# A three-stage kernel in float32: loads and preparatory work of its first stage rearranged, and its dense stage cut into blocks of 384 tokens

## The reference

```python
# 1: gated linear attention; 4 batches, 8 heads, 768 tokens, head size 48
for t in range(S):
    state = alpha[:, :, t, :, None] * state + np.einsum('bhd,bhe->bhde', k[:, :, t], v[:, :, t])
    y[:, :, t] = np.einsum('bhd,bhde->bhe', q[:, :, t], state)
# 2: each of 3072 tokens goes to the best of 8 experts
logits = (x / (norm(x) + 1e-6)) @ (emb / (norm(emb) + 1e-6)).T / tau
out[mask] = gate_w[mask, None] * (np.maximum(x[mask] @ w1[e], 0.0) @ w2[e])   # 384 -> 1024 -> 384
# 3: dense mixture; every token goes through all 4 experts
p = domain_probs / (domain_probs.sum(-1, keepdims=True) + 1e-9)
for e in range(4):
    out += p[:, e:e + 1] * (np.maximum(x @ w1[e], 0.0) @ w2[e])               # 384 -> 1024 -> 384
```

## Time and profile before

| what | value |
|---|---|
| time, median of 3 runs | 1276.92 us (1276.18 to 1277.35) |
| the profiled execution: its time, its span | 1278.89 us, 1277.2 us |
| TensorE busy | 1210.4 us, 95% of the span |
| VectorE, ScalarE, GpSimd busy | 504.4, 397.4, 153.2 us |
| moved by DMA | 102.86 MB |
| granted TensorE clock, mean over the span | 0.976 |

### The profile page before, as it was taken

One profiled execution on the slowest core, in us unless ns is written; L12 is line 12 of the kernel. 1 busy time (PEld: TensorE's weight loads), 2 busy tenths in 40 slices (PEclk: granted clock), 3 DMA queues, 4 the chain that ended last, 5 costly groups with the idle time before them and its releaser, 6 DMA issues.

```text
span 1277.2 us, 20420 instructions
## 1 busy us (share of the span) xinstructions
PE 1210.4 (95%) x7357; PEld 1089.5 (85%) x7358; DVE 504.4 (39%) x833; ACT 397.4 (31%) x765; POOL 153.2 (12%) x184
## 2 busy tenths in 40 slices
PE   4999559999999879999999999999999999999998
PEld 4898439989989859999999999988888899999997
DVE  5999763443444242232233233234334224223321
ACT  5667414554544331121122122123222112112111
POOL 3455522232232100000000000000000000000000
PEclk9999769999999879999999999999999999999999
DMA  8777222344244233011011011011001101300000
GB/s 302 258 249 256 74 78 87 135 142 142 86 164 169 75 130 99 26 50 50 1 50 49 0 49 49 0 50 51 1 1 50 50 1 50 123 0 0 25 25 25
DMA packets 50964, 102.86 MB, mean 81 GB/s; under 512 B 7184, under 2 KB 32784, under 8 KB 50784
## 3 DMA queue, kind: packets, MB, share of 16 engines
q1 hardware_dynamic: 42304, 84.28, 19.2%
q0 software_dynamic: 3520, 10.82, 2.7%
q10 hardware_dynamic: 5088, 7.08, 1.6%
HBM read 87.42 MB, written 14.75 MB: 80 GB/s over the span
## 4 chain that ended last, share of the span: by engine, by line
PE 91%; DVE 3%; DMA 2%; issue 1%; ACT 1%; SPq 1%; POOL 0%; ACTq 0%; DVEq 0%; POOLq 0%
PE bank L763 11%; PE bank L765 11%; PE bank L764 11%; PE bank L778 10%; PE bank L780 10%; PE bank L779 10%; PE bank L672 3%; PE bank L684 3%; PE bank L686 3%; PE bank L685 3%; PE bank L674 3%; PE bank L673 3%; PE bank L695 2%; PE bank L580 1%; PE bank L563 1%; PE bank L589 1%
## 5 line engine op out<-in xcount | busy, mean ns | idle before, releaser
L997 ACT ACTIVATE act_hi<-bank 128x512 fp32r<-128x512 f32 x192 | 114.9, 598 | 583.6 <-PE bank L765 583.6
L778 PE MATMUL bank<-w_hi,act_hi 128*128 128x384 f32 x768 | 258.5, 337 | 0.0
L780 PE MATMUL bank<-w_hi,act_lo 128*128 128x384 f32 x768 | 258.1, 336 | 0.0
L779 PE MATMUL bank<-w_lo,act_hi 128*128 128x384 f32 x768 | 258.1, 336 | 0.0
L763 PE MATMUL bank<-xt_hi,w_hi 128*128 128x512 f32 x576 | 228.2, 396 | 2.9 <-DVE xt_lo L1419 2.9
L764 PE MATMUL bank<-xt_lo,w_hi 128*128 128x512 f32 x576 | 227.8, 396 | 0.0
L765 PE MATMUL bank<-xt_hi,w_lo 128*128 128x512 f32 x576 | 227.8, 395 | 0.0
L1446 DVE SCALAR_TENSOR_TENSOR act_lo<-bank,act_hi 128x512 fp32r<-128x512 f32 x192 | 132.2, 689 | 163.8 <-ACT act_hi L997 163.8
L778 PEld LDWEIGHTS bank<-w_hi,act_hi 128*128 128x128 f32 x768 | 144.4, 188 | 1.1
L779 PEld LDWEIGHTS bank<-w_lo,act_hi 128*128 128x128 f32 x768 | 144.4, 188 | 0.9
L780 PEld LDWEIGHTS bank<-w_hi,act_lo 128*128 128x128 f32 x768 | 144.4, 188 | 0.0
(11 more groups left out here) (188 smaller groups left out, 1359.6 us busy)
## 6 DMA issues: line engine op xcount, KB each, us to landing
inputs<-qka SPq DMA_DIRECT2D x24, 512.0 KB, 4.0
w_raw<-w1a SPq DMA_DIRECT2D x8, 1536.0 KB, 6.9
w_raw<-w2a SPq DMA_DIRECT2D x8, 1536.0 KB, 6.5
w_raw<-w1b SPq DMA_DIRECT2D x8, 1536.0 KB, 6.4
w_raw<-w2b SPq DMA_DIRECT2D x8, 1536.0 KB, 6.6
inputs<-gated SPq DMA_DIRECT2D x24, 256.5 KB, 2.7
vin<-v SPq DMA_DIRECT2D x24, 256.0 KB, 4.2
x_rows<-x_sb ACTq DMA_DIRECT2D x24, 192.0 KB, 2.3
```

The lines of the kernel that those rows point to most:

```text
L778: pe.matmul(o, act_hi[:, f, r], w2_hi[:, f, :], start=(f == 0), stop=False)
L779: pe.matmul(o, act_hi[:, f, r], w2_lo[:, f, :], start=False, stop=False)
L780: last = pe.matmul(o, act_lo[:, f, r], w2_hi[:, f, :], start=False, stop=(f == FT - 1))
L997: act.activation(act_hi[:, f, :], d_h[f % BANKS][:, :], ACT.Relu).then_inc(dh_hi, 1)
```

## The change

1. **Loads.** `first` comes first. Of each batch gates and `qka` go ahead, `v` one batch later and under a semaphore of its own (`v_ready`), so that GpSimd no longer waits for it. The load of `emb_sb` leaves the normal path. The first w1, w2 and `probs` move from behind the first loads to behind the four loads of chunk 1.
2. **Embedding squares.** VectorE squares the small table that `turn` already holds, TensorE sums it over the partitions with a matrix of ones in step 3 (`p_emb`), and the root on ScalarE moves to step 5. Eight squares and sums leave ScalarE.
3. **36 transposes of the identity** into an unused bank, ahead of TensorE's first scores.
4. **VectorE order.** `mask(0)` before `decay(2)`; the constant memsets first. `prepare` is split: `constants` behind steps 2, 4 and 5, the root of the embedding norms behind step 20, the shares behind step 21.
5. **Steps.** Seven are written out ahead of the loop instead of three, and the loop has three turns instead of four.
6. **Dense blocks** of 384 tokens: four per half instead of three, SUB 3 instead of 4, three `d_y` banks.

```diff
-BLK = 512
+BLK = 384
...
-        d_h, d_y = bank[0:4], bank[4:8]
+        d_h, d_y = bank[0:4], bank[4:4 + SUB]
...
-        PEEL, TURNS = 3, 4
+        PEEL, TURNS = 7, 3
...
-            load(0, 0)
             sp.dma_start(gate0[:, :, :], first).then_inc(first_loaded, 16)
-            load(1, 0)
-            sp.dma_start(emb_sb[:, :, :].rearrange("p e d -> p (e d)"),
-                         emb.rearrange("(o e) d -> o (e d)", o=1).to_broadcast([P, E1 * MODEL])).then_inc(emb_loaded, 16)
-            load(2, 0)
-            load(3, 0)
+            for b in range(B):
+                sp.dma_start(inp[b][:, 2 * W:3 * W + 1], gated[b, 0]).then_inc(gates_loaded[b], 16)
+                sp.dma_start(inp[b][:, 0:2 * W], qka[b, 0, :, 0:2 * W]).then_inc(in_ready[b], 16)
+                if b >= 1:
+                    sp.dma_start(vin[b - 1][:, :], v[b - 1, 0]).then_inc(v_ready[b - 1], 16)
...
                     load(b, c + 1)
+                if c == 0:
+                    sp.dma_start(w1_raw[:, :, :], w1a[0].rearrange("(k p) f -> p k f", p=P)).then_inc(w1_loaded, 16)
+                    sp.dma_start(w2_raw[:, :, :], w2a[0].rearrange("(g p) n -> p g n", p=P)).then_inc(w2_loaded, 16)
+                    sp.dma_start(pw[:, :, :], probs.rearrange("(n p) e -> p n e", p=P)).then_inc(pw_loaded, 16)
...
+                if least == 3:
+                    pe.wait_ge(emb_squared, 1)
+                    pe.matmul(p_emb, ones_f[:, :], emb_sq[:, :, :].rearrange("p a e -> p (a e)"), start=True, stop=True)
...
             pe.wait_ge(consts, CONSTS)
+            for _ in range(WARM):
+                pe.transpose(p_warm, ident[:, :], ident[:, :])
             front(0, 0, 0)
...
+                if least in (2, 4, 5):
+                    constants(least)
+                if least == STEPS - 4:
+                    prepare()
                 if least == STEPS - 3:
-                    prepare()
+                    shares()
...
+            def constants(part):
+                if part == 2:
+                    dve.wait_ge(const_loaded, 32)
+                    dve.tensor_tensor(emb_sq[:, :, :], turn[:, :, 2 * D:XW], turn[:, :, 2 * D:XW],
+                                      ALU.mult).then_inc(emb_squared, 1)
+                    dve.tensor_copy(iota_f[:, :, :], iota_i[:, :, :]).then_inc(prep_order, prep.one())
+                    dve.tensor_copy(iota_b[:, :, :], iota_i[:, :, :]).then_inc(prep_order, prep.one())
+                elif part == 4:
+                    dve.tensor_copy(token_row[:, :], token_row_i[:, :]).then_inc(prep_order, prep.one())
+                    dve.tensor_copy(token_tile[:, :, 0], tile_no_i[:, :]).then_inc(prep_order, prep.one())
+                    dve.tensor_copy(spare[:, :], spare_i[:, :]).then_inc(prep_order, prep.one())
+                else:
+                    dve.wait_ge(prep_order, prep.now())
+                    dve.tensor_scalar(rank_w[:, 0, :], iota_f[:, 0, 0:E1], -1.0, float(E1),
+                                      ALU.mult, ALU.add).then_inc(prep_order, prep.one())
+                    dve.tensor_scalar(limits[:, 0, :], iota_f[:, 0, 0:NT], float(P), None,
+                                      ALU.mult).then_inc(prep_order, prep.one())
+                    dve.reciprocal(tau_sb[:, :], tau_sb[:, :]).then_inc(prep_order, prep.one())
...
-                            pe.matmul(o[:, :], w1_hi[:, k, w], xt_hi[:, k, cols], start=(k == 0), stop=False)
+                            pe.matmul(o[:, 0:BLK], w1_hi[:, k, w], xt_hi[:, k, cols], start=(k == 0), stop=False)
```

More of the change, by code:

```diff
@@ L206, in build @@
         pool_order = sem("pool_order")
+        v_ready = [sem(f"v_ready{b}") for b in range(B)]
         emb_squared = sem("emb_squared")
+        emb_known = sem("emb_known")
         emb_root = sem("emb_root")
@@ L288, in build @@
         CONSTS = 10
+        WARM = 36
         BANKS = 4
@@ L435, in _ @@
                         steps = half * E2 * HB + (E2 - 1) * HB + t
-                        sp.wait_ge(dy_used, BANKS + steps * SUB + s + tiles)
+                        sp.wait_ge(dy_used, SUB + steps * SUB + s + tiles)
                         n = half * HT + t * SUB + s
@@ L582, in turn_x, with outputs @@
                 last.then_inc(x_ready, 1)
-            def outputs(n, b, least):
+            def outputs(n, b, c, least):
                 j = least % 2
@@ L1093, in update @@
                                   dstate[b][:, :, :], ALU.add).then_inc(delta_used, 1)
+            dve.memset(ones_b[:, :], 1.0)
+            dve.memset(ones_f[:, :], 1.0).then_inc(dve_order, own.one())
             decay(0, 0, 0, 0)
@@ L1097, in _ @@
             decay(1, 1, 0, 1)
-            dve.memset(ones_b[:, :], 1.0)
-            dve.memset(ones_f[:, :], 1.0).then_inc(dve_order, own.one())
+            mask(0, 0)
             decay(2, 2, 0, 2)
-            mask(0, 0)
             ahead, each = own.n, 4
@@ L1445, in expert @@
                                 last.then_inc(w2_split, 1)
-                        dve.scalar_tensor_tensor(out=act_lo[:, f, :], in0=d_h[f % BANKS][:, :], scalar=0.0,
+                        dve.scalar_tensor_tensor(out=act_lo[:, f, :], in0=d_h[f % BANKS][:, 0:BLK], scalar=0.0,
                                                  in1=act_hi[:, f, :].bitcast(F32), op0=ALU.max, op1=ALU.subtract
```

56 lines of the change are left out of this document (26 added, 30 removed).

## The result

The changed kernel takes 1282.27 us (median of 9 runs, 1280.86 to 1286.7) against 1277.35 before (median of 9): ratio 1.0040, 95% interval 1.0024 to 1.0055. It is **slower by 0.4%**; 1272.5 was forecast, with a range up to 1279.5. The profiled execution took 1286.5 (span 1284.8), the one before 1278.89 (1277.2). It is one of two among the nine with a mean granted clock of 0.971; the other seven, at 0.975 to 0.977, took 1280.86 to 1282.85, so its trace shows some 4 us more than a usual run has. The 7.6 us between the two traces divide as follows; the stretches end at the start of the last `logit` reduction, at the first transposes of the dense stage, and at the end of the span.

The account below looks back on a forecast made before the run. TensorE's pace was taken to bound attention after the early transfer waits, and matmuls the dense stage. Attention +0.9 and dense -5.3 gave -4.4 from 1276.9: 1272.5 us, range 1265 to 1279.5.

Parts of the forecast that it names:

- Dense stream: Dense stage: first product's 384-wide matmuls start every 0.1733 us like the second's; 403.1 us becomes 399.4, -3.7 us.
- D: Dense stage: first product's 384-wide matmul misses the second's pace; from 0.1764 us on, slower by over 0.2%; chance 0.04.
- F: Dense stage: a first-product column costs at 384 what it costs at 512 or slightly more; 1276.2 to 1277.8 us; chance 0.05.
- Dense edges, -1.6: Dense stage: smaller blocks have one tile less to prepare and to finish at the edges, saving 1.6 us.
- Start: Start of attention: gates land earlier, decay(4) at 21.5 instead of 30.79, lead 9.3 us; constants then cost some of it.
- The weights in the queue: Attention: 4.2 MB at 333 GB/s take 12.6 us ahead of decay(8), which starts at 48.3, not 44; lead 3.0 us.
- Rival E: Attention: weights come at 246 GB/s instead of 333, 17.1 us instead of 12.6; total 1278.4 us; chance 0.08.
- Clock: Attention: TensorE stands some 6 us at the queue's stall and then runs slower, costing 1.1 us (0 to 2.5).
- Root and masks: End of attention: four root operations wait for GpSimd ahead of mask(22); last logits at T0 + 22.3, +0.4 us.
- T0: End of decay(23), from which the end of attention is counted; 128.97 us in the kernel before.

Follow-up runs that it names:

- e2: Changed kernel with dense blocks back at 512, so the attention part of the change alone: 1283.96 us, ratio 1.0057 to the kernel before.
- e1: Kernel before with only the dense blocks of 384 added: 1272.87 us, ratio 0.9984 to the kernel before.
- e7: Changed kernel with only the load of probs moved, behind the last load of all: 1281.11 us, ratio 1.0028 to the kernel before.
- e4: Changed kernel with the root of the embedding norms and the shares moved behind mask(23): 1276.07 us, ratio 0.9990 to the kernel before.
- e5: Changed kernel with the root moved behind mask(22), ahead of the shares and mask(23): 1281.91 us, ratio 1.0036 to the kernel before.
- e9: Changed kernel with ten more idle transposes behind the turn of each half's first dense block: 1281.10 us, ratio 1.0033 to the kernel before.
- e15: Changed kernel with the table emb_sq declared last: 1282.08 us, ratio 1.0032 to the kernel before.
- e13: Kernel before with only the unused table emb_sq added, ahead of the routed stage's operands: 1279.72 us, ratio 1.0010 to the kernel before.
- e8: Changed kernel with w1 and w2 loaded in parts between other loads, probs last, and root and shares behind mask(23): 1265.97 us, ratio 0.9906.
- e16: Kernel e8 with the table emb_sq declared last: 1265.48 us, ratio 0.9904 to the kernel before.

## Why the prediction was wrong, step by step

The profile was forecast at 1274.5 us and took 1286.5. Of the 12.0 us between them, 2.9 are attention (+3.8 for +0.9), 3.0 the routed stage (+3.0 for 0) and 6.1 the dense stage (+0.8 for -5.3). By the ratios, which don't hang on one run, it is the attention part that went most wrong: +7.3 (e2) for +0.9, and the dense blocks -2.0 (e1) for -5.3.

- **Dense stream**: right. 0.1733 forecast, 0.1733 measured, for the operand pair that no row had shown. Rivals D and F fell. The Trainium skill's advice to keep all dimensions at 512 or more ("TensorE: Matmul & The Clock Gate", Why this matters for your kernels) is given there for reaching 85% of peak; for the width of a single matmul, to which the prediction put it, this trace shows no loss at 384: 0.451 ns a column, against 0.456 at 512.
- **Dense edges, -1.6**: wrong. Where the clock stays up the stage gains 2 to 3.7 us in all, which is the stream's 3.7 at best. The smaller first and last block do give what was forecast (a half's start 2.7 instead of 3.2 us, the last accumulations 1.67 instead of 2.19). It goes again in a third block per half that is turned in the middle of another (from the last matmul ahead of it to the first behind, 6 x 1.08 us instead of 4 x 1.40) and in a longer wait ahead of the second half's turn (1.35 instead of 0.70; e1 1.77). And in six of fourteen traces the clock falls there, which costs about 3.5 us. No case had that.
- **Start**: right in mechanism, nearly in size. `decay(0)` 4.20 (4.2), `decay(4)` 22.14 (21.5), `decay(6)` 34.76 (33.5); VectorE is free for `decay(8)` at 45.3 (44). The constants of step 2 cost 2.49 us (2.4) and of step 4 1.14 (1.1). Those of step 5 cost 1.19 where 2.4 stood, since one of the two operations waited (1.12) and the other did not (0.17).
- **The weights in the queue: this is the step that failed.** "`decay(8)` starts at 48.3": it waits as forecast, but until 52.87 (52.3 to 54.1 in the six other traces with this order of loads). The last load before the weights was issued at 34.64, not 33 (+1.6). `probs` is not in the sum of 4.2 MB at all, and costs 1.8 us by its 3072 packets (e7). The other 1.1 are not the rate: in e7 the engines moved 380 GB/s from 38.43 to 52.12, above the 333 of the sum, but that is 5.2 MB and not 4.2, for the stores of `x_rows` (0.39 MB) and loads issued behind the gates went at the same time. Rival E was nearest in time (1278.4, chance 0.08), for another reason, a slower queue, and the measured 1282.3 is beyond it.
- **Clock**: right in size. The standstill was priced at 1.1 us (0 to 2.5). Between `decay(9)` and the end of `decay(23)` the changed kernel's trace loses 1.8, with the clock at its half level for 10.2 us (54.1 to 64.3); five more traces with the same order of work up to there (e2, e4, e5, e9, e15) lose 0.4 to 1.7, with 6.8 to 10.2 us at that level. So it is the landing that puts `decay(9)` 2.7 us behind the kernel before, and most of the 4.5 at the end of `decay(23)`, where 0.5 was forecast.
- **Root and masks**: right. Four waits; `mask(22)` starts at T0 + 7.2 (7.4 forecast), the last logits at T0 + 21.1 (22.3 forecast, 21.9 before). e4 shows what the place costs: 7 us.
- **Left out altogether**: the routed stage, +3.0 in the trace. It was put at nothing because its code is untouched, but the new table moves its operands, which costs 1.6 us from the first tile to the last (e13, e15). Of the rest, 0.5 lies ahead of the first tile and 0.9 behind the last one's start: a longer wait ahead of the last tile (3.79 against 2.66), a longer one for the rows (8.94 against 7.88), and the clock around them. What decides those stays open; traces of kernels that leave this stage alone differ there by 3.8 us (e1).

What stays open is what decides, from run to run and from kernel to kernel, whether the clock falls around the last routed tile and at the second half; a few us hang on it, and it is why no single trace here gives the change's price.

## What to carry to other kernels

A large load that nobody needs soon goes between small loads in pieces, never as one block ahead of loads that a pipeline waits for; count small packets by number, not by bytes. Work that waits on a shared resource belongs behind the last operation that the bound engine waits for: the same root costs 7 us ahead of the masks, and behind them the last logits come where they were forecast without it (e4; with the weights spread as well, e8, the kernel takes 1265.97 us, 0.9906). When a lead gained early is handed to a wait later, price the clock that the bound engine loses in that wait too, and when a tile is added, look at where it moves the others. Before dividing a profile's difference among causes, see whether the profiled run is a usual one.

## What the runs showed of the hardware

- A table of 128 bytes per partition declared ahead of matmul operands made a routed tile 9.64 to 9.66 us instead of 9.58, in every trace with it (e13: with no other change), and it went when the table was declared last (e15, e16).
- With 3072 packets of 16 bytes (`probs`) outstanding on its queue, the next DMA issue stood 8.35 to 9.80 us in the seven traces of this order; with the same 3 MB ahead and no such packets it took 0.50 (e7). The 48 KB went at a mean of 96 GB/s with what else was moved, where 407 were moved without them.
- While GpSimd runs its operations, a VectorE instruction with two inputs in SBUF, with a scalar, or a cast, ends only when one of them does, whatever its size: 2.27 us for eight elements. (A cast of a single column was not held up, 0.15 us at 42.77.) A mask, with one of its two inputs in PSUM, is not held up (2 in 1.27 us at 140.69, with GpSimd busy from 136.11 to 143.05). The Trainium skill ("SBUF — State Buffer", Who interferes with whom) calls it a lock held for a whole instruction; the trace agrees.
